# A fused attention and MLP kernel: the gate's two halves on ScalarE and VectorE, a slot later, and VectorE's attention split around the gate

## What is computed

```python
for t in range(S):                       # B, H, S, D = 4, 8, 768, 48
    cur = einsum('bhd,bhe->bhde', u * k[t], v[t])
    y[t] = einsum('bhd,bhde->bhe', r[t], state + cur)
    state = w[t][..., None] * state + einsum('bhd,bhe->bhde', k[t], v[t])
...
h = x @ w_in                             # x: 3072 x 384, w_in: 384 x 2048
g = h * np.cos(h)
out = g @ w_out                          # w_out: 2048 x 384
```

## Time and profile before

| What | Value |
|---|---|
| Runs | 727.37, 728.81, 729.34 us; median 728.81 |
| Profiled execution | 730.38 us, its span 728.7 us |
| TensorE busy | 606.3 us (83%), weight loads 528.6 us (73%) |
| VectorE busy | 508.6 us (70%), 1297 instructions |
| ScalarE busy | 320.5 us (44%) |
| GpSimd busy | 219.3 us (30%) |
| Chain that ended last | TensorE 55%, VectorE 23%, ScalarE 8%, DMA 4%, GpSimd 2% |
| Granted TensorE clock, mean | 0.97 |

### The profile page before, as it was taken

One profiled execution on the slowest core, in us unless ns is written; L12 is line 12 of the kernel. 1 busy time (PEld: TensorE's weight loads), 2 busy tenths in 40 slices (PEclk: granted clock), 3 DMA queues, 4 the chain that ended last, 5 costly groups with the idle time before them and its releaser, 6 DMA issues.

```text
span 728.7 us, 12462 instructions
## 1 busy us (share of the span) xinstructions
PE 606.3 (83%) x4549; PEld 528.6 (73%) x4549; DVE 508.6 (70%) x1297; ACT 320.5 (44%) x693; POOL 219.3 (30%) x193
## 2 busy tenths in 40 slices
PE   0534899979997999899989998999899999985972
PEld 0424798969886888788878887888788899872332
DVE  5793889498949794989588957895798654444203
ACT  1522444544464546453645364446443745532012
POOL 4540242234224422433143324332424223220000
PEclk9998899999999999999999999999999999995987
DMA  9742204310431042204120402140310047049836
GB/s 329 301 151 72 80 3 152 104 50 2 152 103 50 2 152 80 74 3 153 40 91 23 152 15 90 49 134 23 102 50 18 2 152 298 0 164 404 276 109 260
DMA packets 39495, 81.39 MB, mean 112 GB/s; under 512 B 3968, under 2 KB 20480, under 8 KB 39424
## 3 DMA queue, kind: packets, MB, share of 16 engines
q1 hardware_dynamic: 39424, 80.48, 31.5%
HBM read 71.02 MB, written 4.72 MB: 104 GB/s over the span
## 4 chain that ended last, share of the span: by engine, by line
PE 55%; DVE 23%; ACT 8%; issue 5%; DMA 4%; POOL 2%; SPq 1%; DVEq 0%; ACTq 0%; POOLq 0%
PE yb L768 20%; PE hb L755 17%; PE ab L681 4%; DVE zs L938 4%; PE ab L700 3%; PE ab L706 3%; DVE ang L1086 3%; DMA w<-w_dram 3%; DVE r_end L974 2%; DVE ang L1094 2%; DVE A L985 2%; PE ab L719 2%; PE pb L778 1%; DVE tmp L952 1%; ACT turns L566 1%
## 5 line engine op out<-in xcount | busy, mean ns | idle before, releaser
L483 POOL TENSOR_TENSOR g_lo<-ang,g_hi 128x384 fp32r<-128x384 f32 x128 | 129.2, 1010 | 402.8 <-DVE g_hi L1099 402.8
L755 PE MATMUL hb<-x_hi,win_hi 128*128 128x384 f32 x384 | 132.1, 344 | 25.2 <-DVE ang L1094 18.5
L768 PE MATMUL yb<-wout_hi,g_hi 128*128 128x384 f32 x384 | 139.2, 362 | 2.4 <-POOL g_lo L483 2.4
L572 ACT ACTIVATE ang<-ang 128x384 f32<-128x384 f32 x128 | 67.3, 525 | 164.8 <-DVE ang L1086 164.7
L755 PE MATMUL hb<-x_hi,win_lo 128*128 128x384 f32 x384 | 130.0, 339 | 0.0
L755 PE MATMUL hb<-x_lo,win_hi 128*128 128x384 f32 x384 | 129.6, 338 | 0.0
L768 PE MATMUL yb<-wout_hi,g_lo 128*128 128x384 f32 x384 | 129.2, 336 | 0.0
L768 PE MATMUL yb<-wout_lo,g_hi 128*128 128x384 f32 x384 | 128.8, 335 | 0.0
L566 ACT ACTIVATE turns<-hb 128x384 int32<-128x384 f32 x128 | 62.7, 490 | 117.4 <-PE hb L755 117.4
L1086 DVE SCALAR_TENSOR_TENSOR ang<-turns,hb 128x384 f32<-128x384 int32 x128 | 70.6, 552 | 61.8 <-ACT turns L566 61.2
L1094 DVE SCALAR_TENSOR_TENSOR ang<-ang,hb 128x384 f32<-128x384 f32 x128 | 69.9, 546 | 46.6 <-ACT ang L574 46.6
(11 more groups left out here) (155 smaller groups left out, 809.1 us busy)
## 6 DMA issues: line engine op xcount, KB each, us to landing
w<-w_dram SPq DMA_DIRECT2D x16, 1536.0 KB, 13.6
zs<-zs_dram SPq DMA_DIRECT2D x16, 384.0 KB, 3.4
zp<-zp_dram SPq DMA_DIRECT2D x16, 384.0 KB, 3.8
kT<-k_by_channel_dram SPq DMA_DIRECT2D x16, 384.0 KB, 5.0
rT<-r_by_channel_dram SPq DMA_DIRECT2D x16, 384.0 KB, 6.0
r_tok<-r_by_token_dram SPq DMA_DIRECT2D x16, 288.0 KB, 5.5
k_tok<-k_by_token_dram SPq DMA_DIRECT2D x16, 288.0 KB, 6.1
v_tok<-v_by_token_dram SPq DMA_DIRECT2D x16, 288.0 KB, 6.3
```

The costliest lines, as they stand in the source:

```text
L483: g.tensor_tensor(g_lo[f % RING][:, :], ang[f % 2][:, :], g_hi[f % RING][:, :].bitcast(F32), ALU.subtract).then_inc(glo_done, 1)
L572: a.activation(ang[f % 2][:, :], ang[f % 2][:, :], ACT.Sin, scale=0.5).then_inc(sin_done, 1)
L755: last = t.matmul(hb[f % 2][:, 0:TT], w[:, k, f * P:(f + 1) * P], x[:, k, :], start=(n == 0), stop=(n == 3 * DK - 1))
L768: last = t.matmul(yb[c][:, 0:DM], gx[f % RING][:, c * P:(c + 1) * P], w[:, f, :], start=(f == 0 and n == 0), stop=(f == NF - 1 and n == 2))
```

## The change

The high half of gate f is cast on ScalarE (`high_half`) in slot f + 1 (HI_LAG = 1), between turns and sine; the low half is subtracted on VectorE (`low_half`) in slot f + 1, ahead of gate f + 1. GpSimd has no MLP work any more. VectorE's attention is cut in two: `attention_first` runs ahead of the gate, `attention_second` behind it. The maximum over zp moves from step 1 to step 0, the first four scaled identities and the r_end product are ahead of the gate, the scans, the other identities and the masked copies behind it. The six suffix scans become one of 768 columns, with `ends` as wide, a one at each chunk's last column. No instruction of TensorE or SyncE is moved.

```diff
+HI_LAG = 1
...
-        ends = sb("ends", [P, P], where=body)
+        ends = sb("ends", [P, COLS], where=body)
...
 # GpSimd
-            def mlp(T, slot):
-                if slot < NF:
-                    f = slot
-                    wait(pool, ghi_done, T, NF, f + 1)
-
-                    wait(pool, y_step, T, NF, f + 1 - RING)
-                    g.tensor_tensor(g_lo[f % RING][:, :], ang[f % 2][:, :], g_hi[f % RING][:, :].bitcast(F32),
-                                    ALU.subtract).then_inc(glo_done, 1)
...
 # ScalarE
+            def high_half(T, f):
+                if 0 <= f < NF:
+                    wait(act, g_done, T, NF, f + 1)
+
+                    wait(act, y_step, T, NF, f + 1 - RING)
+                    a.copy(g_hi[f % RING][:, :], ang[f % 2][:, :]).then_inc(ghi_done, 1)
...
                     if mid is not None:
                         mlp(mid, slot)
+                    if slot < HI_LAG and late is not None:
+                        high_half(late, NF + slot - HI_LAG)
+                    if mid is not None:
+                        high_half(mid, slot - HI_LAG)
                     if att is not None:
                         x_out(att, slot)
...
 # VectorE
-            v.memset(ends[:, P - 1:P], 1.0).then_inc(seeds, 1)
+            v.memset(ends[:, P - 1::P], 1.0).then_inc(seeds, 1)
...
-                    for m in range(CHUNKS):
-                        part = zs[q][:, m * P:(m + 1) * P][:, ::-1]
-                        last = v.tensor_tensor_scan(part, part, ends[:, ::-1], 0.0, ALU.mult, ALU.add)
-                    last.then_inc(suffix_done, 1)
...
+            def attention_second(T, q, step, own):
+                if step == 0:
+                    wait(dve, chain, T, NCHAIN, own[0])
+                    v.tensor_tensor_scan(zs[q][:, ::-1], zs[q][:, ::-1], ends[:, ::-1], 0.0, ALU.mult, ALU.add).then_inc(suffix_done, 1)
...
+            def low_half(T, f):
+                if 0 <= f < NF:
+                    wait(dve, ghi_done, T, NF, f + 1)
+
+                    wait(dve, y_step, T, NF, f + 1 - RING)
+                    v.tensor_tensor(g_lo[f % RING][:, :], ang[f % 2][:, :], g_hi[f % RING][:, :].bitcast(F32),
+                                    ALU.subtract).then_inc(glo_done, 1)
...
-                    wait(dve, g_done, T, NF, f + 1)
-
-                    wait(dve, y_step, T, NF, f + 1 - RING)
-                    v.tensor_copy(g_hi[f % RING][:, :], ang[f % 2][:, :]).then_inc(ghi_done, 1)
-
...
                     if att is not None:
                         for q in range(QUADS):
-                            attention(att, q, slot - QUAD_SLOT[q], own)
+                            attention_first(att, q, slot - QUAD_SLOT[q], own)
+                    if slot < HI_LAG and late is not None:
+                        low_half(late, NF + slot - HI_LAG)
                     if mid is not None:
+                        low_half(mid, slot - HI_LAG)
                         gate(mid, slot)
+                    if att is not None:
+                        for q in range(QUADS):
+                            attention_second(att, q, slot - QUAD_SLOT[q], own)
```

More of the change, by code:

```diff
@@ L496, in tile_steps @@
                                             weights_part(i, HI).bitcast(F32), ALU.subtract).then_inc(w_lo_pool, 1)
[L497 to L505, removed]
+            tile_steps(0, True)
+            for T in range(1, NT):
+                tile_steps(T)
             pool.wait_ge(post_done, NT)
@@ L925, in nth, with attention_first @@
                 return 1
-            def attention(T, q, step, own):
+            def attention_first(T, q, step, own):
                 if step == 0:
@@ new lines, in attention_first, with diagonal_blocks @@
+                if step == 5:
+                    if not isinstance(T, int) or T:
+                        was_read(dve, T - 1, use_of(q, "a2h1"))
+                    st = state[:, q, 0, :, :]
+                    v.tensor_scalar(st, st, keep[:, 0:1], None, ALU.mult).then_inc(state_done, 1)
+                if step == 6:
+                    next_state(T, q, 2)
+            def diagonal_blocks(T, q, cs):
+                if cs[0] == 0:
+                    if q:
+                        y_made(dve, T, 0)
+                    elif not isinstance(T, int) or T:
+                        y_made(dve, T - 1, 1)
+                wait(dve, diag_done, T, QUADS, q + 1)
+                for c in cs:
+                    for h in range(4):
+                        v.tensor_scalar(A[:, h % 2, c, h // 2, :], ident[:, :], diag[:, c, h:h + 1], None, ALU.mult).then_inc(spread, 1)
@@ new lines, in next_state @@
+            def next_state(T, q, c):
+                if c < CH - 1:
+                    wait(dve, state_done, T, QUADS * 2, q * 2 + c + 1)
+                else:
+                    was_read(dve, T, use_of(q, "a2h0"))
+                    wait(dve, scaled_done, T, QUADS * CH * PAIRS, q * CH * PAIRS + PAIRS)
+                side, col = KV_AT[c]
+                b = bank_of(use_of(q, f"a2h{side}"))
+                for pp in range(PAIRS):
+                    last = v.scalar_tensor_tensor(state[:, q, (c + 1) % CH, pp, :], state[:, q, c, pp, :],
+                                                  ptot[:, pp * CH + c:pp * CH + c + 1],
+                                                  ab[b][:, col + pp * D:col + (pp + 1) * D], ALU.mult, ALU.add)
+                last.then_inc(ab_read[b] if c else state_done, 1)
@@ new lines, in attention_second @@
+            def attention_second(T, q, step, own):
+                if step == 0:
+                    wait(dve, chain, T, NCHAIN, own[0])
+                    v.tensor_tensor_scan(zs[q][:, ::-1], zs[q][:, ::-1], ends[:, ::-1], 0.0, ALU.mult, ALU.add).then_inc(suffix_done, 1)
+                    wait(dve, suffix_done, T, QUADS, q + 1)
+                    v.tensor_tensor(ptot[:, :], zp[q][:, 1::P], zs[q][:, ::P], ALU.mult).then_inc(chain, nth(own))
+                    wait(dve, chain, T, NCHAIN, own[0])
+                    v.tensor_scalar(fine[:, :], ptot[:, :], P_LEAST, None, ALU.is_ge).then_inc(chain, nth(own))
+                if step == 1:
+                    sg = sigma[q]
@@ L975, in attention @@
                 if step == 3:
-                    wait(dve, kr_in[q], T, 32, 32)
-                    wait(dve, chain, T, NCHAIN, own[0])
-                    v.tensor_tensor(r_end[:, :], rT[q][:, :], r_end[:, :], ALU.mult).then_inc(ends_done, 1)
-                    was_read(dve, T, use_of(q, "flag"))
-                    v.tensor_copy(verdict[q][:, :], vsum[:, :]).then_inc(verdict_done, 1)
-                if step in (2, 3):
-                    wait(dve, diag_done, T, QUADS, q + 1)
-                    for c in ((0,), (1, 2))[step - 2]:
-                        for h in range(4):
-                            v.tensor_scalar(A[:, h % 2, c, h // 2, :], ident[:, :], diag[:, c, h:h + 1], None, ALU.mult).then_inc(spread, 1)
+                    diagonal_blocks(T, q, (1, 2))
                 if step in (4, 5):
```

42 lines of the change are left out of this document (12 added, 30 removed).

## The result

The changed kernel takes 768.1 us (median of 4 runs, 765.1 to 772.99) against 728.35 us for the kernel before, a ratio of 1.055 with a 95% interval of 1.049 to 1.062. It is slower by 40 us; 765 had been forecast, in a range of 742 to 787. The profiled execution took 772.99 us, with a span of 771.3, so it is the slowest of the four, 42.6 us above the profiled one before.

A forecast was written before the change was run, and what follows sets the result against it. VectorE was taken to bound a tile's first four slots, TensorE most of the rest. Six steady tiles (31.2), the first (2.7), the last (2.8) and prologue and end (-0.4) summed to +36.3 us on 728.81: 765 us, range 742 to 787.

The forecast's parts named there:

- Tile boundary: Between tiles: down steps 14 and 15 wait for VectorE's late low parts, losing 1.9 and 2.5 us.
- k_end locks fine: Slot 0: GpSimd's k_end product holds VectorE's 128x6 comparison until 13.6; angle 1 starts at 13.7, 3.3 us late.
- Slots 1 to 3: These slots win some time back: slot 1 takes about 3.35 us instead of 4.90, slots 2 and 3 4.05 each.
- the rival without it: GpSimd's moved r_tok products fall beside gate and angle, or the wait is partial: 749 us. Chance 0.24.
- the rule: VectorE's two-SBUF-input elementwise instructions and 128x128 scalings wait for a running GpSimd instruction to end, whole; gate and angle don't.
- Masked copies: Slot 4: the copies now follow sine, square and gate, ending 1.6 us later; TensorE's second group of scores needs their banks.
- Slot 11: Masked copy and state sums now stand behind gate 11: 6.2 us instead of 4.98, +1.2 us a tile.
- Slots 6 to 9: Lower VectorE sums but the same pace on TensorE: 0 change, bounds -0.5 and +0.7.
- second collision: Rival: the next tile's tokens land sooner and GpSimd's products hold slot 9's eight scalings: +3.0 in six tiles, 783 us. Chance 0.14.
- High part on ScalarE costs nothing: 16 casts a tile of about 0.5 us fit ScalarE's wait for the angle in ordinary slots; x_hi comes 0.45 us later.
- The steady tile: Sum of its delays: 4.0 + 1.2 = 5.2 us longer, 80.3 us a tile; six such tiles, 31.2 us.
- TensorE's clock: Rival: new waits of 2 to 3.5 us drop the clock, one slow step a tile: 12 us more, 777 us. Chance 0.05.

The follow-up runs named there:

- e9_kend: Changed kernel, but GpSimd's k_end product waits until VectorE has made the quad's seed (the reciprocal): 773.71 us, ratio 1.061.
- e4_pool: Changed kernel, but GpSimd's r_tok products of the second quad wait for gate 5 of the running tile: 752.13 us, ratio 1.030.
- e2_copies4: Changed kernel, but the masked copies of step 4 stand ahead of the low part and gate of their slot again: 751.18 us, ratio 1.031.
- e6_all: Changed kernel, groups 14 and 15's halves on VectorE, masked copies of steps 4 and 5 and two state sums before the gate, second-quad r_tok products after gate 5: 719.24 us.
- e8_allk: e6_all's kernel, with GpSimd's k_end product also waiting for VectorE's seed: 709.43 us, ratio 0.973 to the kernel before.
- e11_ownall: e8_allk, but all sixteen groups keep cast and low part on VectorE behind their own gate: 748.7 us, ratio 1.028 to the kernel before.
- e12_fill_short: Changed kernel with 8 and 12 thrown-away matmuls in TensorE's two tile-boundary waits, before down 14 and down 15: 756.4 us.
- e1_own: Changed kernel, but groups 14 and 15 keep cast and low part on VectorE behind their own gate: 739.44 us, ratio 1.015.
- e10_fill: Changed kernel with 24 and 36 thrown-away matmuls in TensorE's two tile-boundary waits, before down 14 and down 15: 772.94 us.

## Why the prediction was right, point by point

- *Tile boundary.* Waits of 1.83 and 2.63 us were measured where 1.9 and 2.5 stood; projection 1 ends 12.8 us behind the origin (12.6). This step was right, in place, cause and size.
- *k_end locks fine.* Right as an event (1.80 us for 1.9; angle 1 at 13.4 for 13.7) but wrong as a term: projection 1 alone makes angle 1 as late, and e9_kend shows that a free fine gives nothing in this kernel. In the first tile, which has no boundary, the same edit takes slot 0 from 6.52 to 4.93 us.
- *Slots 1 to 3.* Slot 1 3.10 (3.35), slot 2 3.91, slot 3 5.78 with the lock and 3.88 without (4.05): I had VectorE 0.6 us too slow. The lock on the r_end product and low(2) costs 1.9 us in slot 3 (2.3); the rival without it, which I gave 0.24, is out by e4_pool. One reading behind the rule was off, though the rule holds: at 15.48 us, where the scan of 4.72 us was issued, GpSimd was not multiplying but subtracting, until 18.60, and its product of 3.25 us then ran beside the end of the scan:

```profile
15.18 3.42 POOL L495 TENSOR_TENSOR win_lo<-win_raw,win_hi 128x1536 fp32r<-128x1536 f32 x1 [0.47 <-ACT win_hi L598]
```

- *Masked copies.* From angle 4 to angle 6 the tile loses 0.8 us (0.6); TensorE waits 2.11 us for the copies, and e2_copies4 takes 1.7 us a tile away. The copies end 3.5 us behind the start of angle 4 (3.45).
- *Slot 11.* +1.0 us for 1.2, and e6_all and e8_allk bring it back to 5.41.
- *Slots 6 to 9.* 0 was said; they sum to -0.6 us. No second collision: the next tile's products start at 445.65 us, 0.8 us behind the end of the eight scalings of slot 9 (0.5).
- *High part on ScalarE costs nothing.* Right for TensorE, but not quite "without waits of their own": the casts wait 11.7 us for gates in the whole run, up to 1.67 at once, in slot 3 behind the held low part. The worth of cast and lag together was seen too small (e11_ownall).
- *The steady tile.* Without the clock it takes 78.7 us, where 80.3 was forecast: 3.6 us more than before, not 5.2. Over six tiles my waits were 10 us too large, over the whole run 12 (36.3 for about 25): slots 1 to 3, the lock and slots 6 to 9 each took some 0.4 to 0.6 us less than I had.
- *TensorE's clock.* The rival I gave 0.05 happened, beside the forecast and not in its place, and with it one of my signs of being wrong, a granted clock below 1.00 inside the tiles. I had argued from waits of 2.2 us in a tile that left the clock alone. That was the weight loader's wait; the matmuls' own, which is what compares with the new ones, was 1.92 us at the longest, once in each of the six steady tiles, with none over 1.1 us beside it, and no fall came behind it:

```profile
300.51 0.44 PE L755 MATMUL hb<-x_hi,win_hi 128*128 128x384 f32 x1 [1.92 <-DVE ang L1094]
```

  The new ones of 1.8 and 2.6 us, within 10 us, brought the clock down to its lower level for ten matmuls or so at nine places, and with two falls elsewhere it costs some 18 us in the profiled run. This step failed: the clock was put at nothing in the sum on the strength of one wait a tile, where the change makes two, close together. The Trainium skill, TensorE: Matmul & The Clock Gate, Part 1: The HAM clock gate, says that an idle TensorE falls to 1.2 GHz until it has been busy for a while. The trace of the change agrees, and so does e12_fill_short, where the idle time was cut and most falls went.

So that 765 is within 3 us of 768.1 is luck: two errors cancel, waits too large by some 12 us and a clock term that had been left out, some 18 us in the profiled run and, as an estimate, some 15 at the median (39.8 less the 25 of waits). The direction, the range and the places of the main terms were not luck; the runs show each. A reader should trust the terms more than their sum.

## What to carry to other kernels

When work is moved one slot later in a software pipeline, look first at the tile's boundary: there the next tile's preparation stands ahead of it, and the consumer's order doesn't shift along. Moving only those groups back kept the gain of the lag. With the masked copies ahead of the gate again and the held instructions placed apart, it turned 5.5% slower into 2.7% faster. A lock or wait that is hidden behind a later one costs nothing until the later one is mended, so try such edits again after each mend. And price every new wait of TensorE twice: the idle time, and what the matmuls behind it lose at half clock, 1.5 us a fall here where TensorE bounds the slot, and next to nothing where the slot behind has slack (e1_own). The sum of terms measured one by one is too large where two of them free the same slot (e6_all).

## What was not expected of the hardware

Short waits were enough for TensorE's clock to fall. Stretches at 1.2 GHz, each ten matmuls or so long, came behind waits of 1.83 and 2.63 us (at the last boundary 1.64) at five boundaries of seven; behind the wait of 2.0 to 2.1 us for the copies in two tiles of seven in the changed kernel, and in all six steady tiles of e10_fill; behind 2.81 and 0.42 us in e1_own; and behind 0.99 and 1.34 us at one boundary of seven in e12_fill_short. In the kernel before, one wait of 1.92 us a tile had none behind it in six tiles. So the length of a wait did not tell by itself whether a fall came, and what else decides is open. A fall cost about 1.5 us at a boundary or in slot 5, and 0 to 0.6 in e1_own.

And holding between VectorE and GpSimd is whole and goes both ways: a comparison of 128x6 takes 1.80 us instead of 0.17, a GpSimd product 2.00 instead of 1.41.
